# Attention, token mixing and a gated feed-forward on one core: k and q loaded by used rows, alpha's verdict taken one step later from another PSUM bank

## Time and profile before

| | us |
|---|---|
| median of 3 runs | 534.57 |
| the 3 runs | 532.6, 534.77, 534.57 |
| the profiled execution | 532.05 |
| its span | 530.3 |
| of it, pair steps in VectorE's steady order, 12.32 to 75.26 | 62.94 |
| from there to TensorE's first work on the mixing layer, at 88.63 | 13.37 |
| the rest, 88.63 to 530.3 | 441.67 |

### The profile page before, as it was taken

One profiled execution on the slowest core, in us unless ns is written; L12 is line 12 of the kernel. 1 busy time (PEld: TensorE's weight loads), 2 busy tenths in 40 slices (PEclk: granted clock), 3 DMA queues, 4 the chain that ended last, 5 costly groups with the idle time before them and its releaser, 6 DMA issues.

```text
span 530.3 us, 11805 instructions
## 1 busy us (share of the span) xinstructions
PE 521.7 (98%) x4142; PEld 512.8 (97%) x4142; DVE 441.2 (83%) x801; ACT 287.4 (54%) x607; POOL 72.0 (14%) x65
## 2 busy tenths in 40 slices
PE   7999999999999999999999999999999999999997
PEld 7999888999999999999999999999999999999997
DVE  8999997998886759767786787999888888889874
ACT  4888888765534434444244553555555454545353
POOL 5988983000000000000000000000000000000000
PEclk9999999999999999999999999999999999999999
DMA  8899997476131020211062011202020110201011
GB/s 326 303 328 327 314 340 228 140 229 214 38 104 31 17 70 28 92 30 54 15 210 89 1 45 58 77 2 90 0 89 32 57 55 34 89 0 47 0 46 45
DMA packets 37163, 56.93 MB, mean 107 GB/s; under 512 B 3328, under 2 KB 27392, under 8 KB 37120
## 3 DMA queue, kind: packets, MB, share of 16 engines
q1 hardware_dynamic: 34000, 51.65, 29.3%
q10 hardware_dynamic: 3120, 4.72, 2.5%
HBM read 42.20 MB, written 14.16 MB: 106 GB/s over the span
## 4 chain that ended last, share of the span: by engine, by line
PE 91%; SPq 2%; DMA 2%; issue 2%; ACT 1%; DVE 1%; POOL 0%; ACTq 0%; DVEq 0%
PE y_bank L1474 26%; PE y_bank L1533 19%; PE theta_bank L1520 10%; PE x_bank L1520 10%; PE y_bank L1504 7%; PE theta_bank L1461 7%; PE weighed L1371 4%; PE x_sum L1328 3%; PE x_sum L1343 2%; PE turned L1357 2%; PE x_bank L1449 1%; SPq L731 1%; DMA x_in<-x_scratch 1%; PE turned L1376 1%; PE x_sum L1314 1%
## 5 line engine op out<-in xcount | busy, mean ns | idle before, releaser
L1533 PE MATMUL y_bank<-first_w,z 128*128 128x384 f32 x576 | 109.5, 335 | 0.0
L1533 PEld LDWEIGHTS y_bank<-first_w,z 128*128 128x128 f32 x576 | 101.2, 188 | 0.0
L1474 PE MATMUL y_bank<-first_w,z 128*128 128x384 f32 x432 | 78.0, 337 | 0.1
L1474 PE MATMUL y_bank<-rest_w,z 128*128 128x384 f32 x432 | 76.9, 336 | 0.0
L1474 PEld LDWEIGHTS y_bank<-first_w,z 128*128 128x128 f32 x432 | 74.5, 188 | 0.3 <-issue 0.3
L1474 PEld LDWEIGHTS y_bank<-rest_w,z 128*128 128x128 f32 x432 | 74.7, 188 | 0.0
L1042 ACT ACTIVATE out_rows<-theta_bank 128x386 f32<-128x386 f32 x32 | 15.8, 493 | 50.6 <-PE theta_bank L1520 50.5
L1273 DVE TENSOR_SCALAR x_rows<-out_rows,taps 128x384 f32<-128x384 f32 x64 | 26.8, 419 | 19.5 <-ACT out_rows L1042 19.4
L1461 PE MATMUL theta_bank<-theta_w,x_t 128*128 128x384 f32 x216 | 41.6, 336 | 0.1
L1276 DVE SCALAR_TENSOR_TENSOR x_rows<-out_rows,taps,x_rows 128x384 f32<-128x384 f32 x64 | 39.6, 619 | 2.3
L1280 DVE SCALAR_TENSOR_TENSOR z_full<-out_rows,taps,x_rows 128x384 f32<-128x384 f32 x64 | 39.6, 619 | 2.3
(11 more groups left out here) (126 smaller groups left out, 974.2 us busy)
## 6 DMA issues: line engine op xcount, KB each, us to landing
a_in<-in_a_rows SPq DMA_DIRECT2D x15, 390.0 KB, 5.7
k_in<-in_k_rows SPq DMA_DIRECT2D x15, 384.0 KB, 5.3
q_in<-in_q_rows SPq DMA_DIRECT2D x14, 384.0 KB, 5.2
v_in<-in_v_tokens SPq DMA_DIRECT2D x16, 288.0 KB, 4.7
x_in<-x_scratch SPq DMA_DIRECT2D x24, 192.0 KB, 2.6
y<-x_all SPq DMA_DIRECT2D x7, 576.0 KB, 3.3
u_scratch<-u_sum ACTq DMA_DIRECT2D x6, 576.0 KB, 3.5
u_first<-u_scratch SPq DMA_DIRECT2D x4, 577.5 KB, 4.4
```

The source lines that it names most:

```text
L1474: ins = pe.matmul(y_bank[2 * d + half][:, 0:HALF], z[s % 2][part][zp][:, d * P:(d + 1) * P], mixing_w(part, wp, s)[:, half_tokens(half)], ...
L1533: ins = pe.matmul(out_bank[half][t][:, 0:MODEL], g[k % 4][gp][:, t * P:(t + 1) * P], out_w[wp][f], start=f == 0 and i == 0, stop=f == FF_T ...
```

## The change

1. **Rows.** The host puts the 48 dimensions of a head on the rows `4 * (d // 3) + d % 3` of its slot, so that the unused rows are those with remainder 3 by 4, spread over all 128 partitions. Loads of k and q from pair 2 on are issued as two transfers, of the 64 even rows and of the 32 rows with remainder 1, and leave out the 32 unused ones, which keep the zeros of the first, whole loads. The semaphores count 32 for a pair in place of 16, and SP adds 16 to each for the first loads. Alpha and v are loaded as before.
2. **The bank.** `shortfalls` moves from the bank `turned` to free words of VectorE's `resets` bank. TensorE's `judge` (still in step 14) waits for `before_done(14)`, VectorE's last read of that bank, in place of `by_token(13)`; VectorE's next read, `scan_after(15)`, waits for the small matmul; `added(13)` no longer waits for VectorE.
3. **The place of the verdict.** VectorE's four small operations, now all in `place`, move from step 14 to step 15, behind `scan_before(15)`. `divert` on TensorE and VectorE moves from there to the start of `pair_tail`; TensorE's now waits for `mask_late(14)` too. SP's `decide` stays where it is, in step 14.

```diff
+ROWS_OF_HEAD = [4 * (d // 3) + d % 3 for d in range(HEAD_DIM)]
...
@@ pair_step
         if p == JUDGED_AT:
-            do.divert()
+            do.place()
...
         if i == JUDGED_AT:
             do.judge()
-            do.place()
...
     def pair_tail():
         p, o = PAIRS - 1, PAIRS - 2
+        do.divert()
         do.scan_state(o)
...
-    shortfalls = turned[0:1, ADDED:ADDED + 2 * PAIRS]
+    shortfalls = resets_words[0:1, PACKED // 2:PACKED // 2 + 2 * PAIRS]
...
-    got_k, got_q = ([count(f"got_{x}{u}", 16) for u in range(2)] for x in "kq")
+    got_k, got_q = ([count(f"got_{x}{u}", 32) for u in range(2)] for x in "kq")
...
@@ sync
         def rows(tiles, source, got, n):
-            sp.dma_start(tiles[n % len(tiles)][:, :], source[n, :, :]).then_inc(got[n % len(tiles)].sem, 16)
+            u = n % len(tiles)
+            if n < len(tiles) or tiles is a_in:
+                sp.dma_start(tiles[u][:, :], source[n, :, :]).then_inc(got[u].sem, 16)
+            else:
+                for used in (slice(0, P, 2), slice(1, P, 4)):
+                    sp.dma_start(tiles[u][used, :], source[n, used, :]).then_inc(got[u].sem, 16)
...
+        for got in (got_k, got_q):
+            for t in got:
+                sp.sem_inc(t.sem, 16)
...
@@ vector
         def scan_after(i):
...
+            if i == LAST_PAIR:
+                dve.wait_ge(all_measured, 1)
...
-        def judge():
-            dve.wait_ge(all_measured, 1)
+        def place():
             dve.tensor_reduce(total[:, :], shortfalls, mybir.AxisListType.X, ALU.add).then_inc(judged, 1)
             dve.wait_ge(judged, 1)
             dve.tensor_scalar(in_range[:, :], total[:, :], 0.0, None, ALU.is_le).then_inc(judged, 1)
-
-        def place():
             dve.tensor_scalar(batch_of[LAST][:, :], total[:, :], 0.0, float(LAST), ALU.is_gt, ALU.add).then_inc(judged, 1)
...
@@ tensor
         def added(p):
...
             k_copied.done(pe, p)
-            if p == JUDGED_AT - 1:
-                pe.wait_ge(judged, 1)
...
         def judge():
             measured.done(pe, PAIRS - 1)
             capped.done(pe, PAIRS - 1)
-            k_copied.done(pe, JUDGED_AT - 1)
+            before_done.done(pe, JUDGED_AT)
             pe.matmul(shortfalls, ones[:, :], sums[:, :], start=True, stop=True).then_inc(all_measured, 1)
...
         def divert():
             pe.wait_ge(judged, 2)
-            late_copied.done(pe, JUDGED_AT - 1)
+            late_copied.done(pe, JUDGED_AT)
             by_state.if_out_of_range(pe, in_range, by_state.path_tensor)
...
@@ in_slots
-    out[:, :, 0:HEAD_DIM] = rows.reshape(PAIRS, 2, HEAD_DIM, -1)
+    out[:, :, ROWS_OF_HEAD] = rows.reshape(PAIRS, 2, HEAD_DIM, -1)
```

More of the change, by code:

```diff
@@ L127, in source @@
             if x == "a":
-                return a_rows.rearrange("n (g d) (c s) -> n g d c s", g=2, s=SPAN)[n, g, 0:HEAD_DIM, :, 1:CHUNK + 1]
+                return a_rows.rearrange("n (g d) (c s) -> n g d c s", g=2, s=SPAN)[n, g, :, :, 1:CHUNK + 1]
             if x == "v":
                 return v_rows.rearrange("(n g) d (c t) -> n g d c t", g=2, t=CHUNK)[n, g, :, :, :]
-            return {"k": k_rows, "q": q_rows}[x].rearrange("n (g d) (c t) -> n g d c t", g=2, t=CHUNK)[n, g, 0:HEAD_DIM, :, :]
+            return {"k": k_rows, "q": q_rows}[x].rearrange("n (g d) (c t) -> n g d c t", g=2, t=CHUNK)[n, g, :, :, :]
         def path(sp):
@@ L141, in path @@
                     for g in range(2):
-                        sp.dma_start(self.rows[x][g * SLOT:g * SLOT + HEAD_DIM, :].rearrange("p (c t) -> p c t", t=CHUNK),
+                        used = HEAD_DIM if x == "v" else SLOT
+                        sp.dma_start(self.rows[x][g * SLOT:g * SLOT + used, :].rearrange("p (c t) -> p c t", t=CHUNK),
                                      source(x, n, g)).then_inc(self.got.sem, 16)
@@ L841, in first_pair @@
         def first_pair():
-            for chunks, k_got, q_got, a_done, k, b_done, q in (
-                    (AHEAD, first_k_got, first_q_got, first_after, first_k, first_before, first_q),
-                    (BEHIND, got_k[0].sem, got_q[0].sem, after_done.sem, k_done.sem, before_done.sem, q_done.sem)):
+            for chunks, a_done, k, b_done, q in (
+                    (AHEAD, first_after, first_k, first_before, first_q),
+                    (BEHIND, after_done.sem, k_done.sem, before_done.sem, q_done.sem)):
                 pool.wait_ge(a_done, 1)
-                pool.wait_ge(k_got, 16)
+                if chunks is AHEAD:
+                    pool.wait_ge(first_k_got, 16)
+                else:
+                    got_k[0].done(pool, 0)
                 pool.tensor_tensor(chunked(k_scaled[0][:, :])[:, chunks, :], chunked(k_in[0][:, :])[:, chunks, :],
@@ L850, in first_pair @@
                 pool.wait_ge(b_done, 1)
-                pool.wait_ge(q_got, 16)
+                if chunks is AHEAD:
+                    pool.wait_ge(first_q_got, 16)
+                else:
+                    got_q[0].done(pool, 0)
                 pool.tensor_tensor(chunked(q_scaled[0][:, :])[:, chunks, :], chunked(q_in[0][:, :])[:, chunks, :],
@@ L1304, in _ @@
         dve.wait_ge(dve_const, N_DVE_CONST)
-        program(dve, Work(scan_after=scan_after, scan_before=scan_before, judge=judge, place=place, mask=mask, scan_state=scan_state,
+        program(dve, Work(scan_after=scan_after, scan_before=scan_before, place=place, mask=mask, scan_state=scan_state,
                           divert=divert, lower=lower, angle=angles, fill=fill, product=product, theta_low=theta_low, low=low, round_z=round_z, load_weight=load_weight, sums=sums_of, end=end, spare=spare,
```

## The result

| | kernel before | changed kernel |
|---|---|---|
| median of 16 runs each | 532.76 | 535.38 |
| span of the profiled execution | 530.3 | 533.0 |

The ratio is 1.005, with an interval of 1.0037 to 1.0063: **slower by 2.7 us**, where no change (-0.3 us) was forecast. That 535.38 lies inside the stated range of 531.7 to 536.0 is luck: the upper end was the late x_in, added to a median 1.8 us too high. The ratios leave out two slow runs, one of 2930 us of the kernel before and one of 641 us of g2.

What follows compares the result with a forecast made beforehand. VectorE was taken to bound the pair steps. Loads 0, judgement -0.5 and x_in +0.23 gave -0.3 us, so 534.3 us against a median of 534.57, "the same"; range 531.7 to 536.0.

Steps and rivals of the forecast that it cites:

- the late x_in: Rival at the tail's `added(15)`: x_in takes 4.20 us again, +1.3 us, 535.9 us, still "the same"; chance 0.10.
- The step that failed: SP's queue in pair steps: two added issues of 0.43 us fit its 2.2 us wait before v, costing nothing.
- The step next to it: Split loads of k and q: second half's 0.43 us later start and the 12.5% shorter queue cancel.
- VectorE sets the step: Pair steps, 12.32 to 75.26 us: VectorE bounds each 4.84 us step, so lighter loads gain nothing.
- DMA share near 0.83: Pair steps: transfer engines' busy share falls from 0.95 to about 0.83 with the lighter loads.
- the rival that the queue is not relieved: Transfers' fixed part eats the saved bytes: DMA share stays 0.95, time as forecast; counted within the forecast's 0.61.
- Bytes down by 2.75 MB: Loads from pair 2 on: 28 loads of k and q each shrink from 384 to 288 KB.
- The stage from 88.63: From 88.63 us to the end, TensorE-busy: untouched by the change, moves as a whole, keeps 441.7 us.
- The judgement's sum of -0.3 us: Steps 14 and 15 to `added(15)`: judgement -0.5 us, later x_in +0.23 us, together -0.3 us.
- Slower by the transfer rate: Rival in pair steps: k and q below 245 GB/s take the step from VectorE; half rate +14 us, 549; chance 0.06.
- Runs that wait for data: Rival: slower runs had scans stopped by late loads; lighter loads give back up to -2.8 us, 531.8; chance 0.20.

Runs made afterwards that it cites:

- g2: Changed kernel with k and q loaded whole, plus 20 already met waits on SP behind each such load from pair 2 on: 534.10 us, ratio 1.0021.
- e1: Changed kernel with k and q loaded whole again, one transfer of 128 rows each; bank and verdict place as changed: 532.57 us, ratio 0.9996.
- g1: Changed kernel with q loaded whole again and only k split into 64 and 32 rows: 533.09 us, ratio 0.9999.
- e4: Changed kernel with all rows of k and q loaded, in two strided transfers of 64 even and 64 odd rows: 535.88 us, ratio 1.0071.
- e3: Changed kernel with dimensions on each slot's first rows, k and q in two transfers of 48 adjacent rows: 536.93 us, ratio 1.0083.
- f1: Changed kernel with dimensions on each slot's first rows, later loads of k, q and alpha each one transfer of rows 0 to 111: 538.66 us, ratio 1.0115.
- h1: As g2, changed kernel with whole k and q loads, but with 45 met waits on SP behind each: 542.78 us, ratio 1.0176.
- h2: Changed kernel, k and q split, with alpha's loads issued from ScalarE's queue at the end of its step: 536.32 us, ratio 1.0059.

## Why the prediction was wrong

**The step that failed** is "SP has that much room, and two issues of some 0.43 us each ... take 0.9 of it", by which the loads were put at a cost of nothing. It failed in two ways.

- The bill was too small. A split load costs 1.12 us for two issues, +0.69 us; alpha's issue grew from 0.39 to 0.53 us and each pair of stores from 0.89 to 1.05. By the steps shown, issues take 1.78 us more, over the whole stretch (56.0 - 35.0) / 13 = 1.6 us a step. The 0.43 was the price of a whole, unstrided issue, taken for one of another shape.
- The room was not what it was taken for. The 2.2 us are a mean, and they lie ahead of v alone. 1.6 us is still less than 2.2, and SP does still wait 6.0 us in 5 waits. But whatever stands between v and alpha delays alpha at once, room or none: from v to alpha took 3.94 us in place of 2.30 in the steps shown. And a mean of 0.6 us that is left does not cover the single issues that take longer than their like: from 53.92 on SP's steps are 5.3 to 5.5 us long.

**The step next to it failed with it**: "The second half of a load starts 0.43 us later but behind a queue that is 12.5% shorter ... I take these two as cancelling." Landing did get shorter in the median (alpha 5.6 to 4.6 us over the stretch), but the leaving slipped from step to step by more: alpha of pair 15 left 3.75 us late. And one load is enough: the second half of the k that GpSimd waited for started 0.5 us behind the first and took 6.0 us, longer than the whole load's 5.3.

**What was right.** VectorE sets the step and lighter loads give it nothing: e1 and g1 stand at the kernel before. DMA share near 0.83: 0.86, though with fewer loads issued in the stretch; scaled to full engines the rate fell from 342 to 319 GB/s, so a part of the rival that the queue is not relieved is in it. Bytes down by 2.75 MB: 56.93 to 54.18. The stage from 88.63 keeps its length. The judgement's sum of -0.3 us: e1 shows -0.22 in its trace, which its runs neither confirm nor deny, with the scan 0.81 us behind the mask in place of 0.58, x_in's issue 6.34 us behind the scan (predicted 6.42), and its landing in 2.52 us (predicted 2.6). With late alpha the same path cost 1.66 us more: 13.25 - 11.59.

**Of the loss**, then, in one trace of each kernel: 1.12 us before `mask(13)`, 0.87 of it by a late half of k, 1.66 us by alpha of pair 15 at the judgement, -0.22 us from the change's own second half; 2.56 us. The first part is the less certain one: e1, without split loads, lost 0.63 us in the same place by a slow k.

**The rivals.** Slower by the transfer rate was priced, for a rate of k and q under 245 GB/s. No view gives their rate alone; all transfers of the changed kernel together keep 319 GB/s if full, and e4 with 331 lost as much, so it is not what happened. It did in e3 and f1, at 277 and 272 GB/s over all. Late x_in did not happen. Runs that wait for data: the lighter load gave nothing in any kernel. The slower rival that did happen, SP's queue, was looked at in the prediction and closed as a cost of nothing; the text named the 0.43 us by which a load is late once the cover is gone, and did not follow it to what a late load stops.

**What stays open.** Why single issues take up to 1.7 us longer, and single loads of k 6.0 to 7.6 us, in kernels with and without split loads; why an issue behind a strided one is dearer; why 112 adjacent rows run slower than 128.

## What to carry to other kernels

Cutting a load into two spends the issuing queue's time, so sum that queue's issues per step, with measured prices of the very shape, before and after, and compare with the step: 0.8 us a step more cost nothing here (g1), 1.2 us some 1.1 us in all (g2), 1.6 us 2.7 (the change), 2.8 us 9.7 (h1), with a mean slack of 2.2. Ask also where in the step the slack lies, since it covers nothing that is issued behind it. Look at the wait that the issuing queue itself has in each step: when it shrinks from every step to a few, suspect the queue, whatever the busy share of the transfer engines says. That it stays proves little: h2 kept 17.3 us of it and lost as much as the change. Bytes saved where transfers are hidden are worth nothing, and leaving rows out can lower the rate below what it saves.

## What the runs showed of the hardware

- Issuing two strided transfers of 64 and 32 rows, or of 64 and 64, took 1.12 us of SP's queue, of 48 and 48 adjacent rows 0.90, one whole transfer of 128 rows 0.39 to 0.45. Single issues took 0.3 to 1.7 us longer, in the kernel before and in the changed one. A wait that was already met took about 0.03 us. A store behind a strided load cost 0.52 us in place of 0.45.
- Over the same stretch the transfer engines, scaled to full, moved 342 GB/s with whole loads, 319 with strided parts, 277 with two blocks of 48 rows, and 277 / 1.02 = 272 with one block of 112.
- x_in, 192 KB, landed in 2.5 us when the queue had run empty and in 4.6 us beside other loads, at 85.56 and 85.61.
